# The tail tile's second layer of an expert MLP: upper and lower parts of the activations in one stationary operand

## The reference

```
N, D, E, F = (3072, 512, 8, 1024)
logits = x @ w_gate + modality_bias[modality_id]
e_idx = np.argmax(logits, axis=1)
...
gate_w = probs[np.arange(N), e_idx]
for e in range(E):
    mask = e_idx == e
    h = np.maximum(x[mask] @ w1[e], 0.0)
    out[mask] = gate_w[mask, None] * (h @ w2[e])
```

## Time and profile before

| what | value |
|---|---|
| median of 3 runs | 1059.54 us (1059.52 to 1059.76) |
| the profiled execution | 1059.81 us |
| its span, first to last instruction | 1058.1 us |
| PE busy | 1048.3 us, 99% of the span |
| DVE, ACT, POOL busy | 64%, 44%, 27% |
| granted TensorE clock | 1.000 |

### The profile page before, as it was taken

One profiled execution on the slowest core, in us unless ns is written; L12 is line 12 of the kernel. 1 busy time (PEld: TensorE's weight loads), 2 busy tenths in 40 slices (PEclk: granted clock), 3 DMA queues, 4 the chain that ended last, 5 costly groups with the idle time before them and its releaser, 6 DMA issues.

```text
span 1058.1 us, 18467 instructions
## 1 busy us (share of the span) xinstructions
PE 1048.3 (99%) x5870; PEld 900.8 (85%) x5871; DVE 678.5 (64%) x1503; ACT 468.3 (44%) x975; POOL 283.4 (27%) x374
## 2 busy tenths in 40 slices
PE   8999999999999999999999999999999999999998
PEld 8999999888888888888888887888988998899996
DVE  7899999866687568758857767976852223522222
ACT  6888888755433343343333335335442212422212
POOL 6888888501000000000000000431332222322222
PEclk9999999999999999999999999999999999999999
DMA  6677788525220020002002001002372111311100
GB/s 199 204 214 216 199 255 261 181 80 161 80 80 1 1 69 12 1 0 80 1 1 81 1 1 39 6 22 81 127 267 69 57 37 44 112 51 60 39 20 21
DMA packets 57358, 90.72 MB, mean 86 GB/s; under 512 B 11470, under 2 KB 40526, under 8 KB 57168
## 3 DMA queue, kind: packets, MB, share of 16 engines
q1 hardware_dynamic: 50816, 75.17, 22.4%
q0 software_dynamic: 6208, 14.40, 4.2%
q10 hardware_dynamic: 272, 0.39, 0.2%
HBM read 70.86 MB, written 21.69 MB: 87 GB/s over the span
## 4 chain that ended last, share of the span: by engine, by line
PE 93%; POOL 3%; DMA 1%; issue 1%; DVE 1%; ACT 0%; POOLq 0%; SPq 0%; DVEq 0%; ACTq 0%
PE twin L1845 25%; PE bank L1895 13%; PE twin L1895 13%; PE twin L1967 12%; PE twin L1982 12%; PE bank L1767 6%; PE bank L1746 2%; PE twin L1734 2%; PE twin L1733 2%; PE bank L1774 2%; POOL k_lo L655 1%; PE bank L1933 1%; PE twin L2008 1%; POOL qs L657 1%; PE bank L1784 1%
## 5 line engine op out<-in xcount | busy, mean ns | idle before, releaser
L726 POOL DMA_INDIRECT list_scratch<-entry,slot_i x24 | 26.8, 1117 | 472.2 <-DVE slot_i L1480 460.9
L1845 PE MATMUL twin<-x_hi,w_hi 128*128 128x512 f32 x380 | 151.1, 398 | 0.0
L1845 PE MATMUL twin<-x_hi,w_lo 128*128 128x512 f32 x380 | 150.4, 396 | 0.0
L1845 PE MATMUL twin<-x_lo,w_hi 128*128 128x512 f32 x380 | 150.3, 396 | 0.0
L1967 PE MATMUL twin<-xg_both,w_hi 128*128 128x256 f32 x768 | 140.1, 282 | 0.3 <-DVE xg_both L1506 0.2
L1606 DVE SCALAR_TENSOR_TENSOR g_lo<-twin,g_hi 128x256 fp32r<-128x256 f32 x96 | 40.7, 424 | 145.5 <-ACT g_hi L1036 145.2
L1967 PEld LDWEIGHTS twin<-xg_both,w_hi 128*128 128x128 f32 x768 | 121.9, 188 | 6.9 <-issue 0.7
L1000 ACT ACTIVATE turns<-turns 128x512 f32<-128x512 f32 x96 | 60.8, 633 | 131.9 <-DVE turns L1383 131.9
L1365 DVE CUSTOM_DVE_ANT_0 whole<-y_sb,raw 128x512 f32<-128x512 f32 x160 | 109.9, 687 | 1.9
L992 ACT ACTIVATE turns<-twin 128x512 f32<-128x512 f32 x95 | 56.4, 593 | 117.4 <-PE twin L1845 117.3
L1967 PE MATMUL twin<-xg_both,w_lo 128*128 128x256 f32 x384 | 107.2, 279 | 0.0
(11 more groups left out here) (246 smaller groups left out, 2423.5 us busy)
## 6 DMA issues: line engine op xcount, KB each, us to landing
raw<-w_expert SPq DMA_DIRECT2D x24, 512.0 KB, 4.5
raw_q<-q_twice SPq DMA_DIRECT2D x31, 384.0 KB, 3.8
raw<-w_dense SPq DMA_DIRECT2D x16, 512.0 KB, 4.5
raw_k<-k_twice SPq DMA_DIRECT2D x16, 448.0 KB, 3.8
raw_k<-k_twice SPq DMA_DIRECT2D x16, 416.0 KB, 4.8
v_sb<-v_n SPq DMA_DIRECT2D x16, 384.0 KB, 4.2
xT_scratch<-x_stage SPq DMA_DIRECT2D x16, 384.0 KB, 3.8
x_raw<-xT_scratch SPq DMA_DIRECT2D x6, 1024.0 KB, 5.5
```

The costliest lines, as they stand in the source:

```text
L1845: last = pe.matmul(hidden_bank(c, f)[:, :], a[:, w], b[:, k, :], start=k == 0 and x == 0, stop=k == KD - 1 and x == 2)
```

## The change

The rest `g_lo` is no longer kept in tiles of its own. For each block of 64 rows the upper and the lower part now stand side by side in `g_hi` (`tail_g`, 64 columns upper, 64 columns lower), so that one stationary operand of 128 columns holds both. `tail_down` then takes two matmuls for each `f`, with `w_hi` and with `w_lo`, in place of three. Rows 0 to 63 of the bank sum the upper part's products, rows 64 to 127 the lower part's (its product with `w_lo` included, which the three matmuls left out). The two halves of the bank have to be added: ACT scales rows 64 to 127 into SBUF (`scale_lower`), with the gates that DVE has copied to those partitions (`high_gates`), and DVE scales rows 0 to 63 and adds the other in the same instruction (`scale_tail`).

```
         def tail_g(half, low):
+            return g_hi[half][:, :].rearrange("p (i h n) -> p i h n", h=2, n=TAIL)[:, :, low, :]
...
+            def scale_lower(t):
+                act.wait_ge(e_down_done, FB2 * (t + 1) + 4)
+                act.wait_ge(h_lo_made, FB2 * t + 10)
+                act.activation(tail_part, EY_BANK[0][TAIL:, :], ACT.Copy, scale=high_gates[TAIL:, 0:1]).then_inc(h_hi_made, 1)
...
-                act.activation(g_hi[1][:, 0:TAIL_COLS], tail_sum[1], ACT.Relu).then_inc(h_hi_made, 3)
+                act.activation(tail_g(1, 0), tail_sum[1].rearrange("p (i n) -> p i n", n=TAIL), ACT.Relu).then_inc(h_hi_made, 2)
                 splits(range(4, EP))
                 if alone:
-                    scale_rows(t, TAIL)
+                    scale_lower(t)
                     split_rows(t + 1, ET_BANK)
                 else:
-                    end_tile(t, TAIL)
+                    split_rows(t + 1, ET_BANK)
+                    scale_lower(t)
...
+                def scale_tail():
+                    dve.wait_ge(now_made, 2 * t + 2)
+                    dve.tensor_copy(high_gates[TAIL:, 0:1], now_gates[0:TAIL, 0:1]).then_inc(h_lo_made, 1)
+                    dve.wait_ge(h_hi_made, n + 8)
+                    dve.wait_ge(y_out_free[0], t + 1)
+                    dve.scalar_tensor_tensor(out=y_out[0][0:TAIL], in0=EY_BANK[0][0:TAIL, :], scalar=now_gates[0:TAIL, 0:1],
+                                             in1=tail_part, op0=ALU.mult, op1=ALU.add).then_inc(ey_scaled[0], 1)
...
-                split_rows(t + 1, ET_BANK)
+                if alone:
+                    scale_tail()
+                    split_rows(t + 1, ET_BANK)
+                else:
+                    split_rows(t + 1, ET_BANK)
+                    scale_tail()
...
-                half, at = f // (D // P), f % (D // P) * TAIL
-                for x, (a, b) in enumerate(((g_hi, w_hi), (g_hi, w_lo), (g_lo, w_hi))):
-                    last = pe.matmul(EY_BANK[0][0:TAIL, :], a[half][:, at:at + TAIL], b[:, w], start=f == 0 and x == 0, stop=f == FB2 - 1 and x == 2)
+                half, at = f // (D // P), f % (D // P) * P
+                for x, b in enumerate((w_hi, w_lo)):
+                    last = pe.matmul(EY_BANK[0][:, :], g_hi[half][:, at:at + P], b[:, w], start=f == 0 and x == 0, stop=f == FB2 - 1 and x == 1)
                 last.then_inc(e_down_done, 1)
...
-                pe.wait_ge(h_lo_made, n + 10)
+                pe.wait_ge(h_lo_made, n + 9)
                 for f in range(4, FB2):
```

More of the change, by code:

```diff
@@ L210, in build_program @@
             spare = sb("spare", [P, 1], where=a)
+            high_gates = sb("high_gates", [P, 1], where=a)
             bpart = tmp
@@ L432, in build_program, with tail_g @@
         tail_sum = [y_sb[:, 2 + i, 0:TAIL_COLS] for i in range(2)]
+        tail_part = y_sb[0:TAIL, 2, :]
+        def tail_g(half, low):
+            return g_hi[half][:, :].rearrange("p (i h n) -> p i h n", h=2, n=TAIL)[:, :, low, :]
         T_START, T_END, T_WHOLE, T_EXPERT, T_TILES, T_USED, T_TURNS = 0, 1, 2, 3, 4 * NE + 4, 4 * NE + 5, 4 * NE + 6
@@ L1036, in keep_positive, with scale_rows @@
                 act.activation(h_hi[f % 4], EH_BANK[f % 2][:, 0:TT], ACT.Relu).then_inc(h_hi_made, 1)
-            def scale_rows(t, rows=P):
+            def scale_lower(t):
+                act.wait_ge(e_down_done, FB2 * (t + 1) + 4)
+                act.wait_ge(h_lo_made, FB2 * t + 10)
+                act.activation(tail_part, EY_BANK[0][TAIL:, :], ACT.Copy, scale=high_gates[TAIL:, 0:1]).then_inc(h_hi_made, 1)
+            def scale_rows(t):
                 act.wait_ge(e_down_done, FB2 * (t + 1) + 4)
@@ L1041, in scale_rows, with end_tile @@
                 act.wait_ge(now_made, 2 * t + 2)
-                act.activation(y_out[0][0:rows], EY_BANK[0][0:rows, :], ACT.Copy, scale=now_gates[0:rows, 0:1]).then_inc(ey_scaled[0], 1)
-            def end_tile(t, rows=P):
+                act.activation(y_out[0], EY_BANK[0][:, :], ACT.Copy, scale=now_gates[:, 0:1]).then_inc(ey_scaled[0], 1)
+            def end_tile(t):
                 split_rows(t + 1, ET_BANK)
-                scale_rows(t, rows)
+                scale_rows(t)
             def expert_tile(t, split=None):
@@ L1085, in tail_tile @@
                 act.wait_ge(h_lo_made, n + 3)
-                act.activation(g_hi[0][:, 0:TAIL_COLS], tail_sum[0], ACT.Relu).then_inc(h_hi_made, 3)
+                act.activation(tail_g(0, 0), tail_sum[0].rearrange("p (i n) -> p i n", n=TAIL), ACT.Relu).then_inc(h_hi_made, 3)
                 splits(range(2, 4))
                 act.wait_ge(h_lo_made, n + 8)
-                act.activation(g_hi[1][:, 0:TAIL_COLS], tail_sum[1], ACT.Relu).then_inc(h_hi_made, 3)
+                act.activation(tail_g(1, 0), tail_sum[1].rearrange("p (i n) -> p i n", n=TAIL), ACT.Relu).then_inc(h_hi_made, 2)
                 splits(range(4, EP))
                 if alone:
-                    scale_rows(t, TAIL)
+                    scale_lower(t)
                     split_rows(t + 1, ET_BANK)
                 else:
-                    end_tile(t, TAIL)
+                    split_rows(t + 1, ET_BANK)
+                    scale_lower(t)
             def tiles_of(first, whole_end, last, r, parity):
@@ L1646, in _, with tail_tile @@
             dve.wait_ge(table_made, 1)
-            def tail_tile(t, split=None):
+            def tail_tile(t, split=None, alone=False):
                 n = FB2 * t
@@ L1662, in tail_rest @@
                 def tail_rest(half):
-                    dve.scalar_tensor_tensor(out=g_lo[half][:, 0:TAIL_COLS], in0=tail_sum[half], scalar=0.0,
-                                             in1=g_hi[half][:, 0:TAIL_COLS].bitcast(F32), op0=ALU.max, op1=ALU.subtract).then_inc(h_lo_made, 2)
+                    dve.scalar_tensor_tensor(out=tail_g(half, 1), in0=tail_sum[half].rearrange("p (i n) -> p i n", n=TAIL), scalar=0.0,
+                                             in1=tail_g(half, 0).bitcast(F32), op0=ALU.max, op1=ALU.subtract).then_inc(h_lo_made, 2 - half)
+                def scale_tail():
[5 more added lines that the diff above has]
+                                             in1=tail_part, op0=ALU.mult, op1=ALU.add).then_inc(ey_scaled[0], 1)
                 splits(range(0, 1))
@@ L1676, in tail_tile @@
                 add_halves(1)
-                dve.wait_ge(h_hi_made, n + 8)
+                dve.wait_ge(h_hi_made, n + 7)
                 tail_rest(1)
                 splits(range(3, EP))
-                split_rows(t + 1, ET_BANK)
+                if alone:
[4 more added lines that the diff above has]
+                    scale_tail()
             def tiles_of(first, whole_end, last, r, parity):
@@ L1685, in tiles_of @@
                         with dve.If(first < last):
-                            tail_tile(first, split=(r + 1, 1 - parity))
+                            tail_tile(first, split=(r + 1, 1 - parity), alone=True)
                         with dve.Else():
@@ L1691, in tiles_of @@
                         with dve.If(first < last):
-                            tail_tile(first)
+                            tail_tile(first, alone=True)
                 with dve.Else():
```

## The result

| | before | changed |
|---|---|---|
| median us (22 runs each, same chips) | 1059.80 | 1058.17 |
| lowest to highest us | 1059.39 to 1060.70 | 1057.69 to 1058.76 |
| profiled execution us | 1059.81 | 1058.32 |
| its span us | 1058.1 | 1056.6 |

The changed kernel takes 0.9984 of the time before (95% interval 0.9979 to 0.9990), 1.63 us less. The forecast was 1.43 us less and "within 0.2%". The forecast time of 1058.1 us fits better than the forecast gain, and this is luck: it started from the 1059.54 us of three runs, and the kernel before came out 0.26 us higher in the 22.

A forecast was written before the change was run, and what follows sets the result against it. PE was taken to bound the kernel almost everywhere. PE's 1.15 us gain in the middle tile plus 0.28 us in the last, after the output step, made 1.43 us: 1059.54 to 1058.1 us, range 1057.2 to 1059.2.

The forecast's parts named there:

- The turn 0.23 and 0.20 us earlier: One matmul less in f=0 lets the second half's turn start 0.23 us (middle tile) and 0.20 us (last) earlier.
- f=1 to 3 worth nothing: Three matmuls less per tile behind the turn: the saving of 0.69 us in each tile turns into a wait.
- PE lost 0.1 us: Kernel before, middle tile: without a wait f=4 would have started at 898.20, not 898.30.
- the 0.7 to 0.9 that the prediction named as its sign: Sign in the changed kernel's profile: PE waits 0.7 to 0.9 us before f=4 in both tiles, released by DVE's rest.
- f=4 to 7, 0.92 and 0.93 us: Four matmuls less, all on the path: 0.92 us gained in the middle tile, 0.93 in the last.
- The load of 128 columns: PE's wider stationary load takes 188 ns, not 134, but is hidden under the 0.23 us matmul pitch: no cost taken.
- rival (b): The 128-column loads are exposed on PE: 1.1 us back on the path, 1059.2 us; chance 9%.
- The output step, 0.85 us: DVE's scaled addition behind ACT's scaling: 0.75 us plus 0.10 hand-over, on the path to the end in the last tile.
- The strided writes: Writing `g_hi` with gaps of 64 columns costs nothing; at most 0.1 us a tile.
- The middle tile, where nobody on the path waits: DVE's addition there, 900.98 to 901.73, is over before the next tile's relu at about 901.85, so costs nothing.
- (a): Rival: all 16 matmuls removed from the second layer count, giving 1056.7 us; chance 6%.
- (c): Rival: PE's clock falls from 2.4 to 1.2 GHz behind the waits before f=4, giving 1063.3 us; chance 5%.

The follow-up runs named there:

- e3: Changed kernel with one more matmul in f=0 of the tail tile's second layer, ahead of the second half's turn: 1058.69 us.
- e1: Changed kernel with one more matmul in each of f=1, 2 and 3 of the tail tile's second layer: 1058.22 us, ratio 0.9984.
- e5: Changed kernel with the lower rows' product left out of the output, ACT alone scaling rows 0 to 63 into it: 1058.06 us.
- e2: Changed kernel with one more matmul in each of f=4 to 7 of the tail tile's second layer: 1060.09 us, ratio 1.0001.
- e11: Changed kernel with the next rows' turn on PE moved ahead of the second layer in the last tile too: 1058.16 us.
- e7: Changed kernel with the second half's copy on ACT in place of DVE and its turn ahead of f=0: 1057.81 us, ratio 0.9982.
- e12: Changed kernel with e7's and e5's edits together: ACT copies the second half and alone scales the output; 1057.09 us (8 runs), ratio 0.9974.

## Why the prediction was right, point by point

**The turn 0.23 and 0.20 us earlier.** Right: it follows f=0 by 0.55 us in place of 0.78 in the middle tile, by 0.56 in place of 0.73 in the last (0.17). e3 gives it back. The stretch ahead of it was as good as unchanged: f=0 of the middle tile starts at 895.00 before and 895.07 now.

**f=1 to 3 worth nothing.** Right, and shown by e1.

**f=4.** The step "PE lost 0.1 us", with the chain of 2.52 us from the turn to f=4, was misread. The trace before has a matmul of f=3 at 898.06, one pitch ahead of 898.30: PE was not waiting, the rest had just come in time. Nine matmuls don't take 9 × 0.23, because the first pitch behind the turn is 0.32 us (896.13 to 896.45), and the 0.15 us from the rest to f=4 was PE's own pace and no hand-over. The chain itself takes 2.36 us (895.62 to 897.98) in the middle tile and 2.42 in the last (1046.45 to 1048.87), with 0.06 and 0.13 us for the hand-over to PE. So f=4 gained 0.39 and 0.27 us on f=0, not 0.23 and 0.20, and the wait is 0.5 to 0.6 us, not 0.8, outside the 0.7 to 0.9 that the prediction named as its sign. The prior matmul's start should have been looked up in the earlier trace rows, where it was left out, before a wait was read out of two ends that fell together.

**f=4 to 7, 0.92 and 0.93 us.** Too large: from f=4 to the next work it was 2.02 us in place of 2.76 and 1.98 in place of 2.79, so 0.74 and 0.81. The pitch is 0.23 as forecast, but the first one behind the wait is 0.33 (897.98 to 898.31), and the step into the next tile's first matmul 0.29 in place of 0.23. Neither was in the sum. The 0.33 goes with the late load: in e1, where f=4 comes at full pitch and its load ahead of it, the next matmul follows after 0.23 us. The 0.29 doesn't go with the wait: e1 has none at f=4 and takes 0.35 us there (899.94 to 900.29). Its cause is open.

The two errors nearly cancel: 0.39 + 0.74 = 1.13 us up to the next tile's first matmul, forecast 1.15. Up to the piece of the chain behind the next tile's first hidden blocks (905.59 before, 904.62 after) 1.04 us is left, since that tile's first pitch is longer too (900.00 to 900.33 in place of 901.06 to 901.30). The last tile gained 1.08 us from f=0 to the turn of the next rows (6.04 to 4.96), forecast 1.13. That the sum came out is luck in this part.

**The load of 128 columns.** It takes 188 ns and lies under the 0.23 us pitch wherever matmuls follow each other, so rival (b) with its 1.1 us is out. It is not free where PE comes out of a wait, because there the load starts with its matmul and not one pitch ahead of it. f=0 in the last tile waits in both kernels, before first, then changed (other engines left out):

```profile
1046.86 0.13 PEld L2008 LDWEIGHTS twin<-w_hi,g_hi 128*64 128x64 f32 x1 [1.15 <-issue]
1046.87 0.44 PE L2008 MATMUL twin<-w_hi,g_hi 128*64 128x512 f32 x1 [0.71 <-DVE g_lo L1663]
1047.15 0.39 PE L2008 MATMUL twin<-w_lo,g_hi 128*64 128x512 f32 x1
...
1045.88 0.19 PEld L2032 LDWEIGHTS twin<-w_hi,g_hi 128*128 128x128 f32 x1 [1.18 <-issue]
1045.89 0.49 PE L2032 MATMUL twin<-w_hi,g_hi 128*128 128x512 f32 x1 [0.74 <-DVE g_hi L1674]
1046.22 0.39 PE L2032 MATMUL twin<-w_lo,g_hi 128*128 128x512 f32 x1
```

The first pitch is 0.28 us with a load of 64 columns and 0.33 with one of 128; the difference of 0.05 is the loads' own, 134 and 188 ns. The changed kernel has three such places (this one and f=4 twice), so I estimate from this pair that some 0.15 us of rival (b) came true. It is also why the turn gained 0.17 us here and not 0.23. By the Trainium skill, page "TensorE: Matmul & The Clock Gate", section "LDWEIGHTS (loading the stationary operand)", a load takes its columns divided by 1.2 in ns, 53 ns more for 64 columns more. The trace agrees with that slope (54 ns) and not with the size, 188 ns where the rule gives 107.

**The output step, 0.85 us.** The sum of instruction and hand-over was 0.78: 0.743 us for the addition, 0.04 for the hand-over (1051.13 + 0.68 to 1051.85). The strided writes cost nothing (0.42 to 0.47 us, as before). Here are the two new instructions (columns as in the earlier trace rows):

```profile
L1682 DVE SCALAR_TENSOR_TENSOR late<-twin,gates,y_sb x2: 742/743/744, 900.9 to 1051.8; 64x512 f32<-64x512 f32 x2
...
L1679 DVE COPY high_gates<-gates x2: 147/147/147, 899.3 to 1049.1; 64x1 f32<-64x1 f32 x2
```

The last tile's balance up to POOL's DMA is 1.08 − 0.78 = 0.30 us, forecast 0.28. But "on the path to the end" is not right for all of it. In e5 the step is gone, the DMA starts 0.85 us earlier, and the rows land 0.03 us earlier, because the load of code holds the landing. The prediction had no such bound. It came out all the same because in the changed kernel the two bounds lie close together: the rows would have landed 0.34 to 0.42 us behind their last packet (1055.24) by the pace of e1, e2 and e11, and landed 0.57 us behind it.

**The middle tile, where nobody on the path waits.** Right for this kernel: DVE's addition is over before the next tile's relu starts, and without it (e5) the way to the last tile is 0.09 us shorter (144.65 and 144.74). The relu was put 0.4 us too early (it ends at 902.27, forecast 901.85). In e7, with PE 0.6 us earlier still, the cover is gone, as the prediction had warned.

**Sum.** 1.04 + 0.30 = 1.34 us on the engines, 0.18 us from the last DMA's landing (2.51 to 2.33), which the prediction didn't have, less 0.07 us because the changed kernel came to the middle tile later: 1.45, the span's 1.5. The median gives 1.63.

**Rivals.** (a), all 16 matmuls, is out by e1: the ones in f=1 to 3 are free. (b) is out but for the loads behind a wait. (c), a fall of the clock, did not come: the granted clock is 1.00 from 895 to 901 and from 1045 to 1052, with waits of 0.5 and 0.6 us in these stretches. What the Trainium skill describes on the page "TensorE: Matmul & The Clock Gate", section "HAM oscillation — how this bites in real kernels", has no case in this trace.

## What to carry to other kernels

When work is taken off the engine that bounds a kernel, look at each wait behind it and ask how late the chain of the other engines already is: what lies ahead of such a wait is worth nothing, what lies behind it counts in full. Two things that end at the same moment are to be told apart by the start of the instruction before. And where PE meets the wait at all, the first load of the stationary operand behind it is no longer hidden (0.1 us here for 128 columns); the chain is then the next thing to shorten (e7). At the end of a program, look for what else the last DMA waits for before its start is made earlier: in e5 0.85 us of it was worth 0.03.

## What the runs showed of the hardware that was not expected

- Behind a wait, the first pitch of 128x512 matmuls was 0.28 us with a load of 64 columns and 0.33 with one of 128, in place of 0.23. Right behind four transposes it was 0.31 to 0.32 without any wait, with either width.
- Loads of code go on to the very end of the program. The last 16 KB one took 0.9 to 1.3 us of one DMA queue, and in ten of fourteen traces the output rows landed 1.05 us behind its end, 2.2 to 3.15 us behind their DMA's start.
- After a scaled addition of 64x512, DVE started its next instruction 1.06 us behind the addition's end in e7 though its input had been ready for 0.50 us, and 0.02 us behind its input in e12, where there was no addition.
- The hand-over from ACT's relu to DVE's rest in the second half took 0.10 us before the change and 0.03 after it, and in the one trace that exchanged the semaphore's increments it stayed so.
